# Attention before two MLPs, one core: exp of a score tile in two instructions, and products with v that end behind a turn

## The chip, the core and the metric

The kernel runs on 1 core of one Trainium2 chip. The metric is device time in microseconds (us), the median of 3 runs. TensorE is called PE here, VectorE DVE, ScalarE ACT, GpSimd POOL, and the queue that issues most transfers SP.

## The reference

Three stages follow one another; the change touches the first alone. All inputs are float32.

```python
# attention: q, k, v are (2, 8, 1152, 64)
q_pool = q.reshape(B, H, S // 2, 2, D).mean(axis=3)          # 576 queries a head
scores = scale * q_pool @ k^T                                # 576 x 1152 a head
attn   = exp(scores - max) / (sum + 1e-9)
x      = (attn @ v)  laid out as (1152 tokens, 512)
# first MLP:  h = x @ w_in;  g = P(h) / Q(h);  x = g @ w_out     (512 -> 2048 -> 512)
# second MLP: rms norm, silu(xn @ w_gate) * (xn @ w_val) @ w_out (512 -> 1536 -> 512)
```

## The kernel before, in words

**Pairs and slots.** Attention works on one head of each batch together, a *pair* `h` (8 pairs; the middle six are a loop of three rounds with two pairs each). The 1152 queries of a pair are nine *tiles* of 128 queries against 1152 keys: tiles 0 to 3 of the first batch, tile 4 mixed of both (`MIXED`), tiles 5 to 8 of the second. `pair` on each engine goes over the tiles; what PE does between two turns is called a *slot* here, slot `i` beginning with the turn of tile `i`:

- `turn(i)` (L817): nine 128x128 transposes by matmul of the probabilities, back into the PSUM buffer `sc` of the same tile, in three chunks `c` of 384 keys. It waits for the exp of tile `i` (`exp_done`).
- some `pv` matmuls (L835): the product of transposed probabilities with v, for a *group* of queries (`GROUPS`: g0 of 256 columns, g1 and g2 of 320, g3 of 256). A group takes 18 matmuls, nine key tiles for each of the two halves (high and low part) of the probabilities, `pt_hi` and `pt_lo`. `PV_AT` says which matmuls lie in which slot: (group, first, end). g3 is done in slots 0 and 1 of the next pair.
- `qk(i + 2)` (L809): the scores of the tile after next, two matmuls of 384 columns for each of three chunks, three for the mixed tile (so slot 2 has nine). Each chunk waits until DVE has taken the same chunk of tile `i` out of the buffer (`pt_lo`), since there are two buffers `sc`.

**The other engines, tile by tile.** DVE: three maxima over the chunks of tile `i + 1` (L1211), their minimum with sign (L1213), then three `lo_parts` of tile `i` (L1220), which also free `sc`. ACT: three `hi_parts` of tile `i` (L1039) as the chunks are turned, then exp of tile `i + 1` (L1030) as one instruction over 1152 elements with a sum of each row; the sum comes out by a further instruction (ACTIVATION_READ_ACCUMULATOR), and `exp_done` is counted with it. Behind the exp come, in some slots, the evacuations `o_copy` of a finished group (L1057), `sums_plus` (sum + 1e-9, L1045) in slot 0 for the pair before, and `recip_copy` in slot 3 (L1050). The reciprocal itself is on DVE in slot 2 (L1224), its turn on PE in slot 3 (L842).

**Columns.** `pt` has room for two groups; tile `i` is written into `PT_COL[i]`. `hi_parts` of tiles 0, 2, 5 and 7 open a group's columns anew and wait until the group that was there is multiplied (`pv_done`). In the kernel before, that group has ended at least one slot earlier.

**SP and POOL.** SP takes its transfers in program order: raw k and q of the next pair, `shift` (the outputs `o_sb` of the pair before to `o_part`, L385; waits for all four `o_copy`), in odd pairs `load_first_w` (weights of the first MLP), `rows_of_recip`, raw k, q, v. `o_copy(0)` of a pair waits for that `shift` to have landed. POOL splits q, k and v in high and low parts for the next pair; v of the second batch (`values_hi(1)`, L555) waits for the last group of the pair before.

Of the kernel before, what the change touches and what calls it, by code (L numbers as in the profile page):

```python
# [23 lines left out]
P = 128  # L24
# [54 lines left out]

PV_AT = {0: (3, 0, 9), 1: (3, 9, 18), 2: (0, 0, 3), 3: (0, 3, 9), 4: (0, 9, 18), 5: (1, 0, 9), 6: (1, 9, 18), 7: (2, 0, 9), 8: (2, 9, 18)}  # L80
GROUP_OF = {0: 0, 1: 0, 2: 1, 3: 1, 4: 1, 5: 2, 6: 2, 7: 3, 8: 3}


def build(nc, q, k, q_mixed, v, w_in, w_out, a, b, w_gate, w_val, w_out2, rms_g, out):
# [3 lines left out]
    with top:  # L88
# [18 lines left out]
        rms_bias = sbuf(top, "rms_bias", [P, 1])  # L107
        eps_bias = sbuf(top, "eps_bias", [P, 1])
        g_col = sbuf(top, "g_col", [P, DK])
# [7 lines left out]
        neg_part = sbuf(top, "neg_part", [P, 2, 3])  # L117
        sums = sbuf(top, "sums", [P, 2, TILES])
        sums_eps = sbuf(top, "sums_eps", [P, 2, TILES])
# [223 lines left out]
        def _(sp):  # L343
# [76 lines left out]
            def pair(h, par, n):  # L420

                if is_last(h):
                    mixed_keys(1, h)
                    shift(h - 1, 1 - par, n)
                    load_first_w(n)
                    rows_of_recip(h - 1, 1 - par)
                    last_shift(0)
                    last_rows(0)
                    last_shift(1)
                    last_rows(1)  # L430
                    last_shift(2)
                    load_w(sp, *order[0])
                    last_shift(3)
                    return
# [7 lines left out]
                if not is_first(h):  # L442
                    shift(h - 1, 1 - par, n)
                    if par == 1:
                        load_first_w(n)
                    rows_of_recip(h - 1, 1 - par)
                sp.wait_ge(k_split[1], h * 2 + 2)
# [64 lines left out]
        def _(pool):  # L512
# [5 lines left out]
            nc.gpsimd.memset(exp_bias[:], -Q_SHIFT * LN2).then_inc(consts, 1)  # L518
            nc.gpsimd.memset(eps_bias[:], 1e-9).then_inc(consts, 1)
            nc.gpsimd.memset(rms_bias[:], -0.5 * M_SHIFT * LN2).then_inc(consts, 1)  # L520
# [52 lines left out]
            def split_first_half(h):  # L573

                pool.wait_ge(k_split[1], h * 2)
                values_free(1, h - 1)
                queries_sum(0, h)
                values_hi(1)
                pool.wait_ge(q_split[0], h * 4 + 1)
                values_lo(1, h - 1)  # L580
                queries_hi(0)
                keys_hi(0)
                queries_lo(0, h)
                pool.wait_ge(q_split[0], h * 4 + 4)
                keys_lo(0, h)
# [198 lines left out]
        def _(pe):  # L784
# [27 lines left out]
            def turn(i, h, par):  # L812
                pe.wait_ge(exp_done, h * 9 + (i + 1))
                for c in range(3):
                    for j in range(3):
                        m = 3 * c + j
                        ins = nc.tensor.transpose(sc[par][:, c, P * j:P * j + P], prob[par][:, P * m:P * m + P], ident[:])  # L817
# [27 lines left out]
            def pair(h, par, n):  # L845
                for i in range(TILES):
# [10 lines left out]
                    if is_last(h) and i == 8:  # L857
# [3 lines left out]
                        first_product(0)  # L861
                    if i in (0, 1):
                        if not is_first(h):
                            g, j0, j1 = PV_AT[i]
                            pv(g, h - 1, j0, j1)
                    elif is_first(h) and i <= 4:
                        if i >= 3:
                            pv(0, h, *((0, 8) if i == 3 else (8, 2 * KEY_TILES)))
                    elif is_last(h) and i == 7:
                        pv(2, h, 0, 2 * KEY_TILES)  # L870
                    elif not (is_last(h) and i == 8):
                        g, j0, j1 = PV_AT[i]
                        pv(g, h, j0, j1)
                    if i + 2 < TILES:
# [152 lines left out]
        def _(act):  # L1027
            def exps(i, h, s):
                act.wait_ge(max_done, h * 9 + (i + 1))
                nc.scalar.activation(prob[s][:].rearrange("p (c n) -> p c n", c=3), sc[s][:, :, 0:KBANK], ACT.Exp,  # L1030
                                     bias=neg_max[:, s:s + 1], accum_out=sums[:, (s + i) % 2, i:i + 1]).then_inc(exp_done, 1)

            def hi_parts(i, h, s):
                if i in (0, 2, 5, 7) and not (is_first(h) and i < 5):
                    act.wait_ge(pv_done, h * 4 + (GROUP_OF[i] - 1))
                for c in range(3):
                    act.wait_ge(pt_t, (h * 9 + i) * 3 + c + 1)
                    src = sc[s][:, c, 0:KBANK].rearrange("p (t n) -> p t n", t=3)
                    nc.scalar.activation(pt[0][:, 3 * c:3 * c + 3, PT_COL[i]:PT_COL[i] + P], src, ACT.Copy).then_inc(pt_hi, 1)  # L1039

            def sums_plus(h, par, t0=0, t1=TILES):

                act.wait_ge(consts, 6)
                act.wait_ge(exp_done, h * 9 + t1)
                nc.scalar.activation(sums_eps[:, par, t0:t1], sums[:, par, t0:t1], ACT.Identity, bias=eps_bias[:]).then_inc(sums_done, 1)  # L1045

# [12 lines left out]
            def pair(h, par, n):  # L1059
                for i in range(TILES):  # L1060
# [8 lines left out]
                    if i == 2 and is_first(h):  # L1069
                        act.wait_ge(raw_v[0], 16)  # L1070
                        nc.scalar.activation(v2[0][:, :, 0], vraw[0][:], ACT.Copy).then_inc(v_split[0], 1)
                    if i == 1 and not is_first(h):
                        o_copy(3, h - 1)
                    if i == 0 and not is_first(h):
                        sums_plus(h - 1, 1 - par)
                    if i == 3 and not is_first(h):
                        recip_copy(0, h, 1 - par)
                    if is_last(h) and i in (3, 7):
                        sums_plus(h, par, *(SUMMED[0:2] if i == 3 else SUMMED[1:3]))
                    if is_last(h) and i == 8:  # L1080
                        recip_copy(PAIRS, PAIRS + 1, 2, *SUMMED[1:3])
                    for g in {4: [0], 6: [1], 8: [] if is_last(h) else [2]}.get(i, []):
                        o_copy(g, h)
# [44 lines left out]
            act.wait_ge(coefs, 3)  # L1128
            act.wait_ge(consts, 6)
            def square(t):  # L1130
# [73 lines left out]
        def _(dve):  # L1204
# [10 lines left out]
            def lo_parts(i, h, s):  # L1215
                for c in range(3):
# [3 lines left out]
                    nc.vector.tensor_tensor(pt[1][:, kt, col], src, pt[0][:, kt, col].bitcast(F32), ALU.subtract).then_inc(pt_lo, 1)  # L1220

            def recips(count, par, t0=0, t1=TILES):
                dve.wait_ge(sums_done, count)
# [9 lines left out]
            def pair(h, par, n):  # L1233
                for i in range(TILES):
# [195 lines left out]
```

## Time and profile before

| | us |
|---|---|
| median of 3 runs | 683.77 (683.64 to 684.41) |
| the profiled execution | 684.07 |
| its span in the trace | 682.3 |
| attention in that span | up to about 244 |
| one pair in steady state, turn of tile 0 to turn of tile 0 | 29.3 |

The page gives, for each engine, the busy time over the whole span. The three stages have different limits, so that shares of the span say little on the change; the rows below are read inside one steady pair (70.50 to 99.80 us). The starts of PE matmuls, not their durations, show its pace, because matmuls overlap. The granted clock of TensorE is at its full level (1.00) in every stretch.

### The profile page before, as it was taken

The numbers are of one execution on the slowest core, as the hardware profiler recorded it, in microseconds if no ns is written. First come the engines' busy times: TensorE is split into PE (matmuls) and PEld (weight loads), VectorE is DVE, ScalarE is ACT, GpSimd is POOL, SyncE is SP. The second block draws the span as 40 slices with busy tenths as digits, with TensorE's granted clock in tenths as the row PEclk, the third lists the DMA queues.
The fourth block names the chain that finished last, engine by engine and source line by source line (L and its number), as shares of the span: only waits on it lengthen the run. The fifth ranks groups of instructions, "written<-read, shape, count | busy, mean of one in ns | idle before, by whom it ended". The sixth has DMA issues, their size and how long they took to land.

```text
span 682.3 us, 11834 instructions
## 1 busy us (share of the span) xinstructions
PE 671.4 (98%) x3940; PEld 624.5 (92%) x3940; DVE 514.2 (75%) x1005; ACT 410.8 (60%) x861; POOL 443.4 (65%) x439
## 2 busy tenths in 40 slices
PE   8999999999999999999999999999999999999998
PEld 6899999999999999889999989899999999999996
DVE  6899999999999957989889889977554444444432
ACT  5777877888787878998888888844511111111110
POOL 5887999998999979999889789845614440000000
PEclk9999999999999999999999999999999999999999
DMA  8667467665655420101110110132111100000012
GB/s 219 198 168 203 129 178 227 181 191 149 197 150 150 114 90 0 62 24 39 62 62 5 59 62 18 45 107 80 61 63 62 62 0 1 1 0 1 1 61 78
DMA packets 26012, 60.76 MB, mean 89 GB/s; under 512 B 3304, under 2 KB 7920, under 8 KB 25840
## 3 DMA queue, kind: packets, MB, share of 16 engines
q1 hardware_dynamic: 25680, 59.87, 29.7%
q8 instruction: 25, 0.41, 0.3%
q10 hardware_dynamic: 288, 0.33, 0.2%
q14 instruction: 19, 0.16, 0.1%
HBM read 43.78 MB, written 2.40 MB: 68 GB/s over the span
## 4 chain that ended last, share of the span: by engine, by line
PE 85%; POOL 5%; DVE 4%; ACT 2%; issue 2%; DMA 1%; SPq 0%; DVEq 0%; POOLq 0%; ACTq 0%
PE hb L909 29%; PE ob L966 22%; PE sc L809 11%; PE sc L817 9%; PE misc L835 5%; PE pv_ps L835 5%; PE tb L909 3%; DVE neg_part L1211 1%; POOL num L768 1%; POOL num L766 1%; DMA qrawA<-in_q 1%; DVE pt_lo L1220 0%; ACT num L1107 0%; POOL kqB L595 0%; DVE num L1271 0%
## 5 line engine op out<-in xcount | busy, mean ns | idle before, releaser
L1039 ACT ACTIVATE pt_hi<-sc 128x384 fp32r<-128x384 f32 x216 | 90.4, 492 | 46.3 <-PE sc L817 46.3
L1211 DVE TENSOR_REDUCE neg_part<-sc 128x1 f32<-128x384 f32 x216 | 107.8, 549 | 11.2 <-PE sc L809 9.8
L1220 DVE TENSOR_TENSOR pt_lo<-sc,pt_hi 128x384 fp32r<-128x384 f32 x216 | 106.6, 548 | 2.9 <-ACT pt_hi L1039 1.9
L966 PE MATMUL ob<-wo_hi,gt_hi 128*128 128x512 f32 x252 | 99.6, 395 | 0.5 <-DVE gt_lo L1288 0.5
L966 PE MATMUL ob<-wo_lo,gt_hi 128*128 128x512 f32 x252 | 99.2, 394 | 0.0
L966 PE MATMUL ob<-wo_hi,gt_lo 128*128 128x512 f32 x252 | 99.1, 393 | 0.0
L909 PE MATMUL hb<-xt_hi,wi_hi 128*128 128x384 f32 x280 | 94.8, 339 | 1.0 <-DVE gt_lo L1288 0.7
L909 PE MATMUL hb<-xt_lo,wi_hi 128*128 128x384 f32 x280 | 94.2, 336 | 0.0
L909 PE MATMUL hb<-xt_hi,wi_lo 128*128 128x384 f32 x280 | 94.1, 336 | 0.0
L1030 ACT ACTIVATE prob<-sc,neg_max 128x1152 f32<-128x1152 f32 x72 | 89.1, 1238 | 3.1 <-DVE neg_max L1213 3.1
L817 PE MATMUL sc<-ident,prob 128*128 128x128 f32 x648 | 82.8, 273 | 0.0
L817 PEld LDWEIGHTS sc<-ident,prob 128*128 128x128 f32 x648 | 73.2, 141 | 4.5
L1177 ACT ACTIVATE silu<-hb 128x384 f32<-128x384 f32 x36 | 17.7, 490 | 93.6 <-DVE hb L1364 93.6
L766 POOL TENSOR_TENSOR num<-num,h 128x384 f32<-128x384 f32 x48 | 55.7, 1160 | 16.9 <-ACT lin L1108 16.7
L1185 ACT ACTIVATE gt_hi<-silu 128x384 fp32r<-128x384 f32 x36 | 18.9, 525 | 64.0 <-DVE silu L1369 64.0
L966 PEld LDWEIGHTS ob<-wo_lo,gt_hi 128*128 128x128 f32 x252 | 47.3, 188 | 10.8
L909 PEld LDWEIGHTS hb<-xt_hi,wi_hi 128*128 128x128 f32 x280 | 52.6, 188 | 3.7 <-issue 0.9
L966 PEld LDWEIGHTS ob<-wo_hi,gt_hi 128*128 128x128 f32 x252 | 47.3, 188 | 9.3 <-DVE gt_lo L1288 0.8
L966 PEld LDWEIGHTS ob<-wo_hi,gt_lo 128*128 128x128 f32 x252 | 47.4, 188 | 8.4
L909 PEld LDWEIGHTS hb<-xt_hi,wi_lo 128*128 128x128 f32 x280 | 52.6, 188 | 1.9
L768 POOL TENSOR_TENSOR num<-num,lin 128x384 f32<-128x384 f32 x48 | 50.4, 1050 | 3.8
L909 PEld LDWEIGHTS hb<-xt_lo,wi_hi 128*128 128x128 f32 x280 | 52.6, 188 | 0.0
(173 smaller groups left out, 1706.1 us busy)
## 6 DMA issues: line engine op xcount, KB each, us to landing
wraw<-in_moe_w_out SPq DMA_DIRECT2D x6, 1024.0 KB, 5.0
krawB<-in_k SPq DMA_DIRECT2D x8, 576.0 KB, 4.4
qrawB<-in_q SPq DMA_DIRECT2D x8, 512.0 KB, 5.7
krawA<-in_k SPq DMA_DIRECT2D x7, 576.0 KB, 4.7
o_part<-o_sb SPq DMA_DIRECT2D x14, 288.0 KB, 4.1
qrawA<-in_q SPq DMA_DIRECT2D x7, 512.0 KB, 6.1
wraw<-in_moe_w_in SPq DMA_DIRECT2D x3, 1024.0 KB, 5.0
wraw<-in_moe_w_gate SPq DMA_DIRECT2D x3, 1024.0 KB, 5.1
```

The lines of the kernel that those rows point to most:

```text
L766: nc.gpsimd.tensor_tensor(nm[:], nm[:], h2[:], ALU.mult).then_inc(num, 1)
L768: nc.gpsimd.tensor_tensor(nm[:], nm[:], ln[:], ALU.add).then_inc(num, 1)
L809: ins = nc.tensor.matmul(sc[par][:, c, 0:KBANK], lhs, rhs, start=n == 0, stop=n == len(terms) - 1)
L817: ins = nc.tensor.transpose(sc[par][:, c, P * j:P * j + P], prob[par][:, P * m:P * m + P], ident[:])
L835: ins = nc.tensor.matmul(bank[:, 0:n], v2[x][:, kt].rearrange("p a d -> p (a d)"), pt[e][:, kt, GROUP * buf + c0:GROUP * buf + c0 + n], st ...
L909: ins = nc.tensor.matmul(bank[:, 0:BLOCK], w[i][:, d, col], x[j][:, d, BLOCK * nb:BLOCK * nb + BLOCK], start=d == 0 and n == 0, stop=d == ...
L966: ins = nc.tensor.matmul(ob[(m + 1) % 2][:], gt[i][:, f, P * t:P * t + P], wo[c % 2][j][:, f, :], start=f == 0 and n == 0, stop=f == CHUNK ...
L1030: nc.scalar.activation(prob[s][:].rearrange("p (c n) -> p c n", c=3), sc[s][:, :, 0:KBANK], ACT.Exp, bias=neg_max[:, s:s + 1], accum_out=s ...
L1039: nc.scalar.activation(pt[0][:, 3 * c:3 * c + 3, PT_COL[i]:PT_COL[i] + P], src, ACT.Copy).then_inc(pt_hi, 1)
L1185: nc.scalar.activation(gt[0][:, f, BLOCK * nb:BLOCK * nb + BLOCK], silu[m % 2], ACT.Copy).then_inc(g_hi, 1)
L1211: nc.vector.tensor_reduce(neg_part[:, s, c:c + 1], sc[s][:, c, 0:KBANK], AX.X, ALU.max, negate=True).then_inc(part_done, 1)
L1220: nc.vector.tensor_tensor(pt[1][:, kt, col], src, pt[0][:, kt, col].bitcast(F32), ALU.subtract).then_inc(pt_lo, 1)
```

## The change

- `exps` becomes two ACT instructions, chunks 0 and 1 (768 elements) and chunk 2 (384), each with a sum of its own and an `exp_done` of its own (`EXP_PARTS`). `turn` waits for the first before chunk 0 and for the second before chunk 2.
- `PV_AT` is a list for each slot now, and groups end in the slot *behind* the turn of the tile that takes their columns: g2 keeps two matmuls for slot 0 of the next pair, g3 three for slot 2, g1 one for slot 7. Products in slots 0 to 8 were 9, 9, 3, 6, 9, 9, 9, 9, 9 and are 8, 9, 5, 8, 8, 9, 8, 9, 8. In `hi_parts` only the last chunk waits for `pv_done` (for tile 5 the first).
- `sums_plus` moves from ACT (slot 0) to DVE (slot 1, behind `lo_parts`), where one instruction adds both sums and 1e-9. The constant `eps_bias` and its memset go.
- `o_copy(2)` moves from slot 8 to slot 0 of the next pair, `o_copy(3)` from slot 1 to slot 2. So `shift` is due later, and `load_first_w` goes ahead of it on SP. On POOL `queries_sum(0)` goes ahead of the wait of `values_free`.

```diff
-PV_AT = {0: (3, 0, 9), 1: (3, 9, 18), 2: (0, 0, 3), 3: (0, 3, 9), 4: (0, 9, 18), 5: (1, 0, 9), 6: (1, 9, 18), 7: (2, 0, 9), 8: (2, 9, 18)}
+PV_AT = {0: ((2, 1, 16, 18), (3, 1, 0, 6)), 1: ((3, 1, 6, 15),), 2: ((3, 1, 15, 18), (0, 0, 0, 2)), 3: ((0, 0, 2, 10),), 4: ((0, 0, 10, 18),),
+         5: ((1, 0, 0, 9),), 6: ((1, 0, 9, 17),), 7: ((1, 0, 17, 18), (2, 0, 0, 8)), 8: ((2, 0, 8, 16),)}
+PV_FIRST = {0: (), 1: (), 2: (), 3: ((0, 0, 0, 8),), 4: ((0, 0, 8, 18),)}
+PV_LAST = {6: ((1, 0, 9, 18),), 7: ((2, 0, 0, 18),), 8: ()}
+EXP_PARTS = ((0, 2), (2, 3))
...
-                    shift(h - 1, 1 - par, n)
                     if par == 1:
                         load_first_w(n)
+                    shift(h - 1, 1 - par, n)
...
                 pool.wait_ge(k_split[1], h * 2)
+                queries_sum(0, h)
                 values_free(1, h - 1)
-                queries_sum(0, h)
...
             def turn(i, h, par):
-                pe.wait_ge(exp_done, h * 9 + (i + 1))
                 for c in range(3):
+                    for part, (c0, _) in enumerate(EXP_PARTS):
+                        if c == c0:
+                            pe.wait_ge(exp_done, h * 18 + (2 * i + part + 1))
...
-                nc.scalar.activation(prob[s][:].rearrange("p (c n) -> p c n", c=3), sc[s][:, :, 0:KBANK], ACT.Exp,
-                                     bias=neg_max[:, s:s + 1], accum_out=sums[:, (s + i) % 2, i:i + 1]).then_inc(exp_done, 1)
+                for part, (c0, c1) in enumerate(EXP_PARTS):
+                    dst = prob[s][:, KBANK * c0:KBANK * c1].rearrange("p (c n) -> p c n", n=KBANK)
+                    nc.scalar.activation(dst, sc[s][:, c0:c1, 0:KBANK], ACT.Exp, bias=neg_max[:, s:s + 1],
+                                         accum_out=sums[:, part, (s + i) % 2, i:i + 1]).then_inc(exp_done, 1)
...
-                if i in (0, 2, 5, 7) and not (is_first(h) and i < 5):
-                    act.wait_ge(pv_done, h * 4 + (GROUP_OF[i] - 1))
                 for c in range(3):
+                    if c == (0 if i == 5 else 2) and i in (0, 2, 5, 7) and not (is_first(h) and i < 5):
+                        act.wait_ge(pv_done, h * 4 + (GROUP_OF[i] - 1))
...
-                    if i == 1 and not is_first(h):
-                        o_copy(3, h - 1)
-                    if i == 0 and not is_first(h):
-                        sums_plus(h - 1, 1 - par)
+                    if i in (0, 2) and not is_first(h):
+                        o_copy(2 if i == 0 else 3, h - 1)
...
+            def sums_plus(h, par, t0=0, t1=TILES):
+
+                dve.wait_ge(exp_done, h * 18 + 2 * t1)
+                nc.vector.scalar_tensor_tensor(out=sums_eps[:, par, t0:t1], in0=sums[:, 0, par, t0:t1], scalar=1e-9,
+                                               in1=sums[:, 1, par, t0:t1], op0=ALU.add, op1=ALU.add).then_inc(sums_done, 1)
...
                     lo_parts(i, h, s)
+                    if i == 1 and not is_first(h):
+                        sums_plus(h - 1, 1 - par)
```

## Rows read from the trace of the kernel before

**Rows 1.** The page, first part: busy us (share of the span) and instructions

```profile
PE 671.4 (98%) x3940; PEld 624.5 (92%) x3940; DVE 514.2 (75%) x1005; ACT 410.8 (60%) x861; POOL 443.4 (65%) x439
```

**Rows 2.** Busy time by window: start:end, us, busy us and instructions of each engine, clock

```profile
core 0: us, PE busy (x) PEld busy (x) DVE busy (x) ACT busy (x) POOL busy (x), PEclk, DMA share, GB/s
70.50:86.30 15.80, 15.60 (x116) 14.62 (x115) 15.34 (x38) 12.97 (x29) 14.77 (x17) 1.00 0.47 134
86.30:99.80 13.50, 13.50 (x97) 13.29 (x97) 12.17 (x30) 10.61 (x23) 13.17 (x7) 1.00 0.70 194
```

**Rows 3.** Timeline of PE: turns of tiles 0, 1, 2, 3, 5, next 0 (start, length)

```profile
70.50 1.14 PE L817 MATMUL sc<-ident,prob 128*128 128x128 f32 x9
...
73.62 1.15 PE L817 MATMUL sc<-ident,prob 128*128 128x128 f32 x9
...
76.72 1.15 PE L817 MATMUL sc<-ident,prob 128*128 128x128 f32 x9
...
80.11 1.14 PE L817 MATMUL sc<-ident,prob 128*128 128x128 f32 x9
...
86.31 1.14 PE L817 MATMUL sc<-ident,prob 128*128 128x128 f32 x9
...
99.80 1.15 PE L817 MATMUL sc<-ident,prob 128*128 128x128 f32 x9
```

**Rows 4.** Timeline of PE: v products and scores in slots 8, 0 and 2

```profile
68.26 0.31 PE L835 MATMUL pv_ps<-pt_hi,v2B 128*128 128x320 f32 x1
...
69.43 1.23 PE L809 MATMUL sc<-kqA 128*128 128x384 f32 x6
...
71.40 0.36 PE L835 MATMUL misc<-pt_hi,v2B 128*128 128x256 f32 x1
71.61 0.28 PE L835 MATMUL misc<-pt_lo,v2B 128*128 128x256 f32 x1
...
72.56 1.22 PE L809 MATMUL sc<-kqA 128*128 128x384 f32 x6
...
78.42 0.44 PE L809 MATMUL sc<-km_hi,qm 128*128 128x384 f32 x1 [0.20 <-DVE pt_lo L1220]
```

**Rows 5.** Timeline of DVE, slots 0 and 2

```profile
69.98 1.49 DVE L1211 TENSOR_REDUCE neg_part<-sc 128x1 f32<-128x384 f32 x3 [0.28 <-PE sc L809]
...
71.58 1.48 DVE L1220 TENSOR_TENSOR pt_lo<-sc,pt_hi 128x384 fp32r<-128x384 f32 x3
...
77.82 1.47 DVE L1220 TENSOR_TENSOR pt_lo<-sc,pt_hi 128x384 fp32r<-128x384 f32 x3
79.21 0.20 DVE L1224 RECIPROCAL recip<-sums_eps 128x9 f32<-128x9 f32 x1
79.33 1.53 DVE L1211 TENSOR_REDUCE neg_part<-sc 128x1 f32<-128x384 f32 x3
```

**Rows 6.** Timeline of ACT, slot 0

```profile
71.03 1.26 ACT L1039 ACTIVATE pt_hi<-sc 128x384 fp32r<-128x384 f32 x3 [0.59 <-PE sc L817]
72.16 1.24 ACT L1030 ACTIVATE prob<-sc,neg_max 128x1152 f32<-128x1152 f32 x1
73.26 0.22 ACT L1030 ACTIVATION_READ_ACCUMULATOR prob<-sc,neg_max 128x1 f32 x1
73.35 0.32 ACT L1045 ACTIVATE sums_eps<-sums,eps_bias 128x9 f32<-128x9 f32 x1
```

**Rows 7.** Groups of ACT instructions by form: count, busy us, mean ns, idle before

```profile
L1039 ACT ACTIVATE pt_hi<-sc 128x384 fp32r<-128x384 f32 x216 | 90.4, 492 | 46.3 <-PE sc L817 46.3
L1030 ACT ACTIVATE prob<-sc,neg_max 128x1152 f32<-128x1152 f32 x72 | 89.1, 1238 | 3.1 <-DVE neg_max L1213 3.1
...
L1057 ACT ACTIVATE o_sb<-pv_ps 128x256 f32<-128x256 f32 x8 | 3.2, 403 | 0.0
L1057 ACT ACTIVATE o_sb<-pv_ps 128x320 f32<-128x320 f32 x7 | 3.2, 457 | 0.0
```

**Rows 8.** Line 385 (`shift`), 14 transfers: issue to landing

```profile
DMA to landing us min/median/max: 3.2/4.1/6.6
```

**Rows 9.** Timeline of POOL behind tile 2's turn

```profile
79.12 0.68 POOL L555 TENSOR_SCALAR v2B<-vrawB 128x576 fp32r<-128x576 f32 x1
```

More of the change, by code:

```diff
@@ L107, in build @@
         rms_bias = sbuf(top, "rms_bias", [P, 1])
-        eps_bias = sbuf(top, "eps_bias", [P, 1])
         g_col = sbuf(top, "g_col", [P, DK])
@@ L117, in build @@
         neg_part = sbuf(top, "neg_part", [P, 2, 3])
-        sums = sbuf(top, "sums", [P, 2, TILES])
+        sums = sbuf(top, "sums", [P, 2, 2, TILES])
         sums_eps = sbuf(top, "sums_eps", [P, 2, TILES])
@@ L423, in pair @@
                     mixed_keys(1, h)
+                    load_first_w(n)
                     shift(h - 1, 1 - par, n)
-                    load_first_w(n)
                     rows_of_recip(h - 1, 1 - par)
@@ L518, in _ @@
             nc.gpsimd.memset(exp_bias[:], -Q_SHIFT * LN2).then_inc(consts, 1)
-            nc.gpsimd.memset(eps_bias[:], 1e-9).then_inc(consts, 1)
             nc.gpsimd.memset(rms_bias[:], -0.5 * M_SHIFT * LN2).then_inc(consts, 1)
@@ L861, in pair @@
                         first_product(0)
[L862 to L873, printed above, removed]
+                    special = PV_FIRST if is_first(h) else PV_LAST if is_last(h) else {}
+                    for g, back, j0, j1 in special.get(i, PV_AT[i]):
+                        pv(g, h - back, j0, j1)
                     if i + 2 < TILES:
@@ L1039, in hi_parts @@
                     nc.scalar.activation(pt[0][:, 3 * c:3 * c + 3, PT_COL[i]:PT_COL[i] + P], src, ACT.Copy).then_inc(pt_hi, 1)
[L1041 to L1045, printed above, removed]
             def recip_copy(n, count, slot, t0=0, t1=TILES):
@@ L1071, in pair @@
                         nc.scalar.activation(v2[0][:, :, 0], vraw[0][:], ACT.Copy).then_inc(v_split[0], 1)
-                    if i == 1 and not is_first(h):
-                        o_copy(3, h - 1)
-                    if i == 0 and not is_first(h):
-                        sums_plus(h - 1, 1 - par)
+                    if i in (0, 2) and not is_first(h):
+                        o_copy(2 if i == 0 else 3, h - 1)
                     if i == 3 and not is_first(h):
                         recip_copy(0, h, 1 - par)
-                    if is_last(h) and i in (3, 7):
-                        sums_plus(h, par, *(SUMMED[0:2] if i == 3 else SUMMED[1:3]))
                     if is_last(h) and i == 8:
                         recip_copy(PAIRS, PAIRS + 1, 2, *SUMMED[1:3])
-                    for g in {4: [0], 6: [1], 8: [] if is_last(h) else [2]}.get(i, []):
+                    for g in {4: [0], 6: [1]}.get(i, []):
                         o_copy(g, h)
@@ L1128, in _ @@
             act.wait_ge(coefs, 3)
-            act.wait_ge(consts, 6)
+            act.wait_ge(consts, 5)
             def square(t):
@@ L1240, in pair @@
                     if is_last(h) and i == 8:
+                        sums_plus(h, par, *SUMMED[1:3])
                         coefficients()
@@ L1246, in pair @@
                     if is_last(h) and i == 4:
+                        sums_plus(h, par, *SUMMED[0:2])
                         recips(PAIRS, par, *SUMMED[0:2])
```

## The prediction, made before the change was run

> **What bounds the kernel now.** First the busy times [rows 1]: PE 98% of the span, DVE 75%, ACT 60%. That is an average over three stages, and the change lives in the first. So next the windows of one steady pair [rows 2]. In the second, slots 5 to 8, PE is busy for all 13.50 us, DVE for 12.17. In the first, slots 0 to 4, PE is busy for 15.60 of 15.80 and DVE for 15.34: two engines near their limit. ACT has room in both.
>
> Then the turns on PE's timeline [rows 3]. Slots 0, 1 and 2 last 3.12, 3.10 and 3.39 us, slots 3 and 4 together 6.20, slots 5 to 8 together 13.49 (3.37 each). The pair takes 29.30.
>
> PE's own pace comes from starts of matmuls [rows 3, 4]. A turn takes 71.40 - 70.50 = 0.90. The first v product behind it takes 0.21, each further one (72.56 - 71.61) / 8 = 0.119 with 256 columns and (69.43 - 68.26) / 8 = 0.146 with 320. Six score matmuls take 73.62 - 72.56 = 1.06. So a slot with nine narrow products needs 0.90 + 0.21 + 8 x 0.119 + 1.06 = 3.12, which is just what slot 0 takes, and one with nine wide products 0.90 + 0.21 + 8 x 0.146 + 1.06 = 3.34 against 3.37. **In seven of nine slots PE has no gap worth closing.** It loses time in slot 2, where its three products are over at 76.72 + 0.90 + 0.21 + 2 x 0.119 = 78.07 and the mixed tile's scores start at 78.42, waiting for DVE's `pt_lo` [rows 4]: 0.35. In slots 3 and 4 its own work is 6.0 (2.88 with six products and the reciprocal's turn, which I count as one more transpose, 0.10 to 0.11; 3.12 with nine) against 6.20: 0.2.
>
> **The exp alone.** Now a turn waits for the whole exp. It starts 73.26 - 72.16 = 1.10 before the read of its sum, and that read takes 0.22 [rows 6]: 1.32, and some 0.05 for the signal. From two copies [rows 7] an element costs (457 - 403) / 64 = 0.84 ns, so the exp's fixed part is 1238 - 0.84 x 1152 = 270 ns: 0.92 us for 768 elements, 0.59 for 384. The other end is the line through the 384-element copy and the exp, 0.97 ns an element: 0.87 and 0.49. I take the first, since fixed parts belong to the operation. With the overlap of 0.14 that the exp shows (1.24 long, next at 1.10) the first part's signal comes at 0.78 + 0.22 = 1.00, or 0.32 earlier than now, the second's at 0.78 + 0.09 + 0.45 + 0.22 = 1.54, later by 0.22, but chunk 2 is turned 0.60 behind chunk 0. ACT is kept for 0.78 + 0.09 + 0.45 + 0.09 = 1.41 instead of 1.19. That 0.22 a tile lies in ACT's idle time before `hi_parts` (0.59 in slot 0). So this edit by itself moves nothing in slots whose turn follows the scores without a gap, and has a little to give in slot 3 only.
>
> The Trainium skill, "ScalarE: Activation LUTs", section "What ACT_TABLE_LOAD costs", gives an activation with a pointer as bias 280 ns and 0.833 ns an element, back-to-back ones overlapping by some 93 ns. By that the parts are 0.92 and 0.60, and the trace agrees at 1152 elements: 1.24.
>
> **Products moved.** Slots 5 to 8 held 36 wide products and hold 34: 2 x 0.146 = 0.29 less. They are PE's alone, DVE has slack there, and slots 6 and 8 at 3.37 - 0.15 = 3.22 stay above what DVE needs for a tile: 1.60 from maxima to `pt_lo` (69.98 to 71.58) and 1.39 on to the next (77.82 to 79.21), 2.99 [rows 5]. So 0.29 a pair is gained in full.
>
> Slots 0 to 4 get those two and lose none of their own. PE alone would need, in slots 0, 1, 2, 3 and 4, 3.03, 3.12, 3.17, 3.12 and 3.01: 15.45 against 15.81 now. But DVE and the latency decide:
> - Slot 0. Two wide products of g2 stand behind the turn; they end at about 0.90 + 0.21 + 0.31 = 1.42 behind the turn's start, with the signal 1.5. The last `hi_parts` chunk would start at 0.53 + 2 x 0.385 = 1.30 [rows 6], so it is 0.2 late, its `pt_lo` chunk hardly (due at 71.58 + 0.93, or 2.01 behind the turn; ready at 2.04). The slot comes to 3.09.
> - ACT then: exp from 1.89, free at 3.30, `o_copy(2)` for 0.37 to 3.67, when `hi_parts` of tile 1 could start at 3.09 + 0.53 = 3.62. A tie: 0 to 0.15 late, I take 0.03.
> - Slot 1. `sums_plus` on DVE: between 0.07 (near nothing beside its neighbours) and 0.25 (its 0.32 on ACT, in full); I take 0.12, what the reciprocal takes between its start and the next maxima [rows 5]. With M0 for the turn of tile 0, `pt_lo` of tile 1 starts at M0 + 3.67 + 0.53 = 4.20 and DVE reaches the next maxima at 4.20 + 1.39 + 0.12 = 5.71. Now it does so at 5.72, held by PE. So it is covered, with nothing left over: each further 0.1 costs 0.1.
> - Slot 2. The mixed scores start when DVE has freed chunk 0, at M0 + 5.72 + 1.60 + 0.60 = M0 + 7.92 as now (0.60: 77.82 to 78.42). The two more products fill the hole. The turn of tile 3 stays at M0 + 9.61.
> - Slots 3 and 4: 3.12 (eight products, no hole) and 3.09, the loop from the turn over `pt_lo` back to the scores' last chunk: 1.08 to `pt_lo` (70.50 to 71.58), 1.48 for its three chunks, 0.06 signal, 0.12 weights, 0.35 for two matmuls. Together 6.21, now 6.20.
>
> So slots 0 to 4 stay at 15.8, and **the whole gain is the 0.29 of slots 5 to 8**.
>
> **What else moves.** `queries_sum(0)` now runs on POOL while g3 ends at about 76.72 + 1.5 = 78.3; v is split at 79.12 [rows 9], so that wait stays covered, by 0.8. `shift` is issued some 3.5 us later (two transfers, behind `load_first_w` in odd pairs). In pair 0 and the last the lists for slots of their own hold as many products as before; the last `sums_plus` and reciprocal lie under 18 products of slot 7. Startup stays: its turns are held by `pt_lo` too. What attention gains, the MLPs pass on, since POOL's first chain there starts from PE's first unit.
>
> **Sum.** Pairs 0 to 6: 7 x 0.29 = 2.05. Less 7 x 0.01 and 6 x 0.03: 1.8. The profiled execution took 684.07 (span 682.3, 1.8 around it), 0.30 above the median. 684.07 - 1.8 = 682.27, and from the median 683.77 - 1.8 = 682.0.
>
> **Rivals.**
> 1. *DVE and ACT take it back.* `sums_plus` at 0.25 costs 0.13 a pair, the late `hi_parts` of tile 1 up to 0.15, a late last chunk in slots 0 and 2 the rest. For it: both engines tie with PE in slot 1. Gain 0 to 1.3: 682.5 to 683.8.
> 2. *PE's floor.* The holes close too: 29.30 - (15.45 + 13.20) = 0.65 a pair, 6 x 0.65 + 0.29 = 4.2, so 679.6; closed in part, 680 to 681. It needs PE's holes to hang on exp. Against it: the row says `pt_lo`. The Trainium skill, "Perfetto Trace Analysis", section "Optimizing Scalar/DVE Operations", says that breaking up instructions of engines that aren't saturated can end bubbles elsewhere sooner; by it the sum would be this rival's, and the trace agrees for slot 3 at most.
> 3. *Slower: `o_copy(0)` waits for `shift`.* `o_copy(3)` ends near M0 + 6.21 + 3.65, so the second transfer is issued at 10.4. ACT comes to `o_copy(0)` at M0 + 12.7 + 3.07 = 15.8. It decides from a landing of 5.4 on; now landings take 3.2 to 6.6, median 4.1 [rows 8]. At 6.6 ACT stalls by 1.2, less 0.24 of slack, and PE has no slack in slot 5: 1.0 a pair. In all four odd pairs that is 4 - 1.8 = 2.2 more: 686.0. Against it: `shift` then follows the raw k, q and weights by 3 us instead of running among them.
>
> **How the numbers follow.** A measurement of this kernel can tell about 0.2%, 1.4 us, from no change. Forecast 60%, its own range 681.2 to 683.0, of which three quarters lie below 682.4; rival 1 22%, rival 2 9%, rival 3 9%. Faster by over 0.2%: 0.45 + 0.09 = 0.54; slower: rival 3 and some mishap, 0.08; the rest, 0.38, within. The range reaches from the near part of rival 2 past the end of rival 1: 680.8 to 684.0.
>
> **What would show it.** Slots 6 and 8 of a steady pair at 3.22, slots 5 and 7 still at 3.37, the pair at 29.0 to 29.1. The mixed scores start 7.9 behind the turn of tile 0, waiting for `pt_lo`, PE's hole there 0.1 instead of 0.35. Exp at 0.92 and 0.59. ACT's idle before `hi_parts` near zero in slot 1. The forecast is wrong if slots 0 to 4 come out away from 15.8 by more than 0.15, or if ACT waits for a transfer in slot 4.

## The result, and the profile after

| | before | after |
|---|---|---|
| median, us | 683.92 (683.64 to 684.41, 4 runs) | 692.99 (692.1 to 693.57, 4 runs) |
| the profiled execution, and its span | 684.07, 682.3 | 692.1, 690.3 |
| first matmul of the first MLP to the last matmul | 244.15 to 678.59: 434.44 | 249.60 to 686.65: 437.04 |

The ratio is 1.0129 [1.0117, 1.0141]: the change costs 1.3% where 0.25% of gain was forecast. The profiled executions differ by 8.0 us, of which 5.45 lie ahead of the first MLP and 2.6 in the MLPs, which the change does not touch. The granted clock is 1.00 in both.

The page after, its first part as in [rows 1]:

```profile
PE 675.1 (98%) x3940; PEld 625.0 (91%) x3940; DVE 515.5 (75%) x1014; ACT 427.5 (62%) x996; POOL 443.3 (64%) x438
```

PE, with as many instructions, is busy for 3.7 us more, and 4.3 us more of the span lie outside its busy time. The groups by form, as in [rows 7]:

```profile
L1027 ACT ACTIVATE prob<-sc,neg_max 128x768 f32<-128x768 f32 x72 | 66.0, 916 | 2.4 <-DVE neg_max L1200 2.4
L1027 ACT ACTIVATE prob<-sc,neg_max 128x384 f32<-128x384 f32 x72 | 43.3, 601 | 0.0
L1212 DVE SCALAR_TENSOR_TENSOR sums_eps<-sums 128x9 f32<-128x9 f32 x7 | 3.7, 534 | 0.0
L1048 ACT ACTIVATE o_sb<-misc 128x320 f32<-128x320 f32 x8 | 3.5, 440 | 9.3 <-PE misc L839 9.3
```

The exp costs ACT 109.3 us instead of 89.1, as forecast. Two of these rows are odd. `sums_plus` takes 534 ns on average for nine elements a row. And ACT stood idle for 9.3 us in front of the copies of 320 columns out of `misc`, where it waited for nothing before:

```profile
L1057 ACT ACTIVATE o_sb<-misc 128x320 f32<-128x320 f32 x8 | 3.7, 458 | 0.0
```

The windows of the pair that [rows 2] shows, slots 0 to 4 and slots 5 to 8 (the columns are the same):

```profile
70.69:86.75 16.06, 15.84 (x118) 15.07 (x117) 15.73 (x39) 14.18 (x39) 15.02 (x18) 1.00 0.44 127
86.75:100.70 13.95, 13.62 (x95) 12.86 (x94) 12.18 (x29) 11.51 (x32) 13.47 (x8) 1.00 0.68 195
```

The second window, PE's own where DVE has slack, grew from 13.50 to 13.95 although it holds two products fewer, and PE has a hole of 0.33 in it. Slot by slot, from the starts of the turns (as in [rows 3]; us, the last column to the next turn of tile 0):

```
slot               0     1     2     3     4     5     6     7     8    pair
before, pair 2   3.11  3.10  3.39  3.05  3.15  3.37  3.37  3.37  3.38  29.30
after,  pair 2   3.15  3.10  3.64  3.09  3.08  3.35  3.22  4.17  3.21  30.01
before, pair 4   3.11  3.11  3.38  3.05  3.14  3.35  3.34  3.37  3.37  29.23
after,  pair 4   3.14  3.11  4.28  3.09  3.08  3.34  3.22  4.17  3.22  30.65
```

Slots 6 and 8 are the 3.22 of the forecast. Slot 7 is 4.17 or 4.18 in each of pairs 0 to 6, and slot 2 is long in pairs 2, 4, 6 and 7 only. PE's timeline of slot 7 of pair 2, from the end of slot 6 to the turn of tile 8 (start, length):

```profile
92.25 1.23 PE L811 MATMUL sc<-kqB 128*128 128x384 f32 x6
93.33 1.14 PE L821 MATMUL sc<-ident,prob 128*128 128x128 f32 x9
94.22 0.39 PE L839 MATMUL misc<-pt_lo,v2A 128*128 128x320 f32 x1
94.45 0.30 PE L839 MATMUL pv_ps<-pt_hi,v2B 128*128 128x320 f32 x1
...
95.47 0.31 PE L839 MATMUL pv_ps<-pt_lo,v2B 128*128 128x320 f32 x1
96.11 1.54 PE L811 MATMUL sc<-kqA 128*128 128x384 f32 x6 [0.33 <-DVE pt_lo L1207]
97.49 1.14 PE L821 MATMUL sc<-ident,prob 128*128 128x128 f32 x9
```

The single product into `misc` behind the turn of tile 7 is g1's last. The scores of slot 7 could have started at 95.62, one step of 0.146 after the last product; they start at 96.11, and then last 1.38 to the next turn instead of 1.06: 0.49 + 0.32 = 0.81, the growth of the slot. PE waits for `pt_lo`; what was late ahead of that is on ACT's timeline (the first two lines are of slot 0, for the comparison further down):

```profile
72.63 0.90 ACT L1027 ACTIVATE prob<-sc,neg_max 128x768 f32<-128x768 f32 x1
...
74.38 0.89 ACT L1036 ACTIVATE pt_hi<-sc 128x384 fp32r<-128x384 f32 x2
...
91.76 0.92 ACT L1027 ACTIVATE prob<-sc,neg_max 128x768 f32<-128x768 f32 x1
...
92.63 0.60 ACT L1027 ACTIVATE prob<-sc,neg_max 128x384 f32<-128x384 f32 x1
...
94.65 0.44 ACT L1048 ACTIVATE o_sb<-misc 128x320 f32<-128x320 f32 x1 [1.32 <-PE misc L839]
94.98 1.25 ACT L1036 ACTIVATE pt_hi<-sc 128x384 fp32r<-128x384 f32 x3
96.09 0.93 ACT L1027 ACTIVATE prob<-sc,neg_max 128x768 f32<-128x768 f32 x1
```

ACT stands still for 1.32 us in front of `o_copy(1)`, which waits for g1's last product. Behind it in ACT's program are the `hi_parts` of tile 7: due 0.53 behind their turn (93.86), they start at 94.98. The `exp` of tile 8 is behind those. The chain of waits (start, length, what), with `issue` and queue steps between, names the same steps in order:

```profile
93.49 0.98 PE sc L821 x9
94.47 0.16 PE misc L839
...
94.65 0.04 ACT o_sb L1048
...
94.99 0.49 ACT pt_hi L1036
...
95.50 0.57 DVE pt_lo L1207
...
96.11 1.54 PE sc L811 x6
```

Among the waits from 20 to 246 us this one stands third, with its count of 7: once in each pair but the last (in total, times, longest).

```profile
ACT pt_hi L1036 <- PE sc L821: 21.3, 44, 1.7
PEld sc L811 <- DVE pt_lo L1207: 10.0, 33, 1.1
ACT o_sb L1048 <- PE misc L839: 9.3, 7, 1.3
```

The second loss is in slots 1 and 2. The timeline of pair 4, all engines:

```profile
135.89 1.30 POOL L661 TENSOR_TENSOR wo_lo<-wout_raw,wo_hi 128x512 fp32r<-128x512 f32 x1
...
136.11 1.11 DVE L1212 SCALAR_TENSOR_TENSOR sums_eps<-sums 128x9 f32<-128x9 f32 x1
...
137.14 1.47 DVE L1198 TENSOR_REDUCE neg_part<-sc 128x1 f32<-128x384 f32 x3
...
139.22 1.42 POOL L561 TENSOR_TENSOR v2B<-vrawB,v2B 128x576 fp32r<-128x576 f32 x1
...
139.33 0.45 PE L811 MATMUL sc<-km_hi,qm 128*128 128x384 f32 x1 [0.87 <-DVE pt_lo L1207]
...
140.12 0.20 DVE L1217 RECIPROCAL recip<-sums_eps 128x9 f32<-128x9 f32 x1
```

`sums_plus`, nine elements a row, takes 1.11 us here, and ends at 137.22 with the POOL instruction beside it (137.19). In pair 2 it takes 0.47, from 76.32, and again ends with the POOL instruction beside it (L659, to 76.78). In pairs 1 and 3 it takes 0.16: in pair 1 POOL runs nothing beside it, in pair 3 a POOL instruction starts at the same moment, 106.33, and runs to 106.81 without holding it. So in these pairs it depends on what POOL has begun when DVE comes. The reciprocal on the same engine, under POOL's L561, takes its usual 0.20. PE is idle for 0.87 ahead of the mixed scores; before it was 0.20, and in pairs 1, 3 and 5, where `sums_plus` takes 0.16, it is not idle there at all.

The sum of the 5.45: slot 7, 7 x 0.80 = 5.6; slots 6 and 8, about -2.0; slots held by `sums_plus`, 0.25 + 0.90 + 0.89 + 0.32 in slot 2 of pairs 2, 4, 6 and 7 and 0.23 in slot 5 of the last, 2.6; the part ahead of pair 1 without its slots 6 to 8, -0.8. Together 5.4. The last term need not be the change's: the turn of tile 0 of pair 1 starts at 41.26 before, but at 40.42 in e2 below, whose attention is the same program.

The third loss is in the MLPs. In PE's timeline of the second MLP, the start of one product of twelve matmuls (`wi`) and of the next (`wv`), both times in the second of its three chunks of weights (the buffers `wi1` and `wv1`), before:

```profile
547.05 0.34 PE L909 MATMUL hb<-xt_hi,wi_hi 128*128 128x384 f32 x1
...
549.13 0.34 PE L909 MATMUL hb<-xt_hi,wv_hi 128*128 128x384 f32 x1
```

and after:

```profile
535.79 0.34 PE L904 MATMUL hb<-xt_hi,wi_hi 128*128 128x384 f32 x1
...
537.91 0.34 PE L904 MATMUL hb<-xt_hi,wv_hi 128*128 128x384 f32 x1
```

Twelve matmuls in 2.08 us and in 2.12, that is 0.1733 and 0.1767 each, without a wait between them. This part of the program is the same in both kernels. What differs is where its buffers lie: `sums` has a second plane (72 bytes a partition more) and `eps_bias` is gone. If buffers are laid out in steps of 32 bytes, all that are allocated behind `sums` lie 32 bytes further on. No run prints an address; the places below are worked out by this rule, and e2, e9 and e12 were built by it and came out as it says.

### The profile page after: what moved, and what is told of

It is laid out like the page before. It is cut to its first block, busy times and chain, and to the rows that moved or that the text cites. A ratio compares the mean times of both kernels' runs of the same rounds, so it can differ in the third digit from the quotient of the medians.

```text
span 690.3 us, 12027 instructions
## 1 busy us (share of the span) xinstructions
PE 675.1 (98%) x3940; PEld 625.0 (91%) x3940; DVE 515.5 (75%) x1014; ACT 427.5 (62%) x996; POOL 443.3 (64%) x438
## 4 chain that ended last, share of the span: by engine, by line
PE 83%; DVE 6%; POOL 5%; ACT 3%; issue 2%; DMA 1%; SPq 0%; ACTq 0%; DVEq 0%; POOLq 0%
PE hb L904 29%; PE ob L961 22%; PE sc L811 11%; PE sc L821 9%; PE misc L839 4%; PE pv_ps L839 4%; PE tb L904 3%; DVE pt_lo L1207 2%; DVE neg_part L1198 2%; POOL num L770 1%; POOL num L768 1%; DMA qrawA<-in_q 1%; ACT pt_hi L1036 0%; ACT num L1094 0%; POOL kqB L597 0%
## 5 line engine op out<-in xcount | busy, mean ns | idle before, releaser
L1036 ACT ACTIVATE pt_hi<-sc 128x384 fp32r<-128x384 f32 x216 | 92.0, 494 | 26.5 <-PE sc L821 22.9
L1027 ACT ACTIVATE prob<-sc,neg_max 128x768 f32<-128x768 f32 (+1 forms) x144 | 106.3, 759 | 2.4 <-DVE neg_max L1200 2.4
L821 PEld LDWEIGHTS sc<-ident,prob 128*128 128x128 f32 x648 | 75.1, 141 | 3.2 <-issue 0.8
```

Of the source, the lines that this page charges most:

```text
L1027: nc.scalar.activation(dst, sc[s][:, c0:c1, 0:KBANK], ACT.Exp, bias=neg_max[:, s:s + 1], accum_out=sums[:, part, (s + i) % 2, i:i + 1]).th ...
```

## The experiments

Three theories were put to the test, each on one of the losses. **A**: `o_copy(1)`, left in ACT's slot 6 while its last product moved into PE's slot 7, holds ACT. **B**: `sums_plus` is held by POOL because it reads two inputs from SBUF; **B2**, formed when that fell: `scalar_tensor_tensor` and `tensor_scalar` from SBUF to SBUF are held, `tensor_reduce` and `reciprocal` are not. **C**: the MLPs' matmuls are slower because of their buffers' addresses; its rival is that the MLPs inherit something from attention's end.

**e1.** The change, with g1's copy in ACT's slot 7.

```diff
-                    for g in {4: [0], 6: [1]}.get(i, []):
+                    for g in {4: [0], (6 if is_last(h) else 7): [1]}.get(i, []):
```

> The changed kernel with one edit: ACT copies group g1 out behind the exp of slot 7 instead of slot 6 (in the last pair, where g1 still ends in slot 6, as it is). Theory A, the copy of g1 stands in front of the matmul that it waits for: slot 7 falls from 4.17 to 3.37 us in all seven pairs, 7 x 0.8 = 5.6 us less, some 687.4 us. Rival, the second exp instruction or the two late matmuls behind the turn make slot 7 long: slot 7 stays above 3.9 and the time at 693.

688.77 (688.56 to 689.48), ratio to before 1.0076 [1.0059, 1.0092]. Slot 7 is 3.34 to 3.37 in pairs 0 to 6, and pairs without a held `sums_plus` take 28.96 to 29.0. ACT's timeline of slots 6 and 7 (the turn of tile 7 of pair 2 is at 92.37, 0.96 earlier than in the changed kernel):

```profile
92.89 1.38 ACT L1036 ACTIVATE pt_hi<-sc 128x384 fp32r<-128x384 f32 x3 [0.52 <-PE sc L821]
94.16 0.90 ACT L1027 ACTIVATE prob<-sc,neg_max 128x768 f32<-128x768 f32 x1
...
95.03 0.58 ACT L1027 ACTIVATE prob<-sc,neg_max 128x384 f32<-128x384 f32 x1
...
95.59 0.44 ACT L1048 ACTIVATE o_sb<-misc 128x320 f32<-128x320 f32 x1
```

`hi_parts` of tile 7 start 0.52 behind the turn, and the copy comes behind the exp without a wait: A is shown. The gain is 4.2 and not 5.6, because the pairs now meet POOL elsewhere: `sums_plus` takes 0.59, 1.24, 0.59 and 0.97 in pairs 4 to 7 and 1.26 behind tile 4 of the last, and slot 2 of these pairs takes 3.78, 4.42, 3.77 and 4.19. In all it costs some 3.4 instead of 2.6. The MLPs take 437.48, 0.4 more. What one loss costs depends on the other.

**e2.** The kernel before, with 32 unused bytes behind `sums`.

```diff
         sums = sbuf(top, "sums", [P, 2, TILES])
+        sbuf(top, "pad", [P, 8])
```

> The kernel before with one unused buffer of 32 bytes behind `sums`, which moves all later SBUF buffers by the 32 bytes by which the change moves them. Theory C, the addresses of the weights set the pace of 384-column matmuls in the MLPs (0.1734 us from one to the next before, 0.1767 after, only where the weights lie in buffers that moved): 2.5 us slower than before, 686.4, with 0.1767 in the products from the second weight buffers. Rival, a drift of that one execution: the time stays at 683.9.

686.13 (685.38 to 686.33), ratio 1.0034 [1.0020, 1.0049], not one instruction changed. The MLPs take 436.75 instead of 434.44, at 0.1767 for the matmuls that took 0.1733. This is C, and it speaks against its rival, since attention is the one of before. In numbers: 432 matmuls on `wv` and as many on `wi1`, up to 0.0034 more each, are up to 2.9 us, and the MLPs took 2.3 more here and 2.6 in the changed kernel.

**e3.** The changed kernel with the same 32 bytes more.

> The changed kernel with 32 unused bytes behind `sums`, so that the later buffers lie 64 bytes from where they lay before. Theory C: the MLPs get their 2.5 us back, 690.5 us. Rival, drift or the number of instructions before the MLPs: 693.

692.31 (692.1 to 692.97), 1.0127 [1.0110, 1.0144]. The matmuls on `wv` are back at 0.1733 to 0.1737 and the MLPs at 435.88, 1.2 less than without the bytes, but `sums_plus` was held in five pairs in this run (slot 2 of 4.28, 3.54, 4.27, 4.29 and 3.67), so that little of it shows in the time.

**e4.** The changed kernel, with one sum read instead of two. The sum over the last 384 keys is left out of the denominator.

```diff
-                nc.vector.scalar_tensor_tensor(out=sums_eps[:, par, t0:t1], in0=sums[:, 0, par, t0:t1], scalar=1e-9,
-                                               in1=sums[:, 1, par, t0:t1], op0=ALU.add, op1=ALU.add).then_inc(sums_done, 1)
+                nc.vector.tensor_scalar(sums_eps[:, par, t0:t1], sums[:, 0, par, t0:t1], 1e-9, None, ALU.add).then_inc(sums_done, 1)
```

> The changed kernel with `sums_plus` on DVE reading only the first sum (one SBUF input instead of two; the sum of the last 384 keys is left out of the denominator). Theory B, the instruction with two SBUF inputs is held while GpSimd has the port (1.11 us instead of 0.16 in pairs 4 and 6, 0.47 in pair 2, 0.58 in pair 7): it takes 0.1 to 0.2 everywhere, slot 2 is 3.39 in all pairs, 2.1 to 2.7 us less, some 690.6. Rival, it waits for the second exp part or for the sums: slot 2 of pairs 4 and 6 stays at 4.27 and the time at 693.

693.45 (692.57 to 693.7), 1.0138 [1.0121, 1.0155]. The timeline of pair 4:

```profile
136.78 1.30 POOL L661 TENSOR_TENSOR wo_lo<-wout_raw,wo_hi 128x512 fp32r<-128x512 f32 x1
...
136.98 1.13 DVE L1212 TENSOR_SCALAR sums_eps<-sums 128x9 f32<-128x9 f32 x1
```

With one input it is held just as long, ending at 138.11 beside POOL's 138.08. B fell as it stood: no second input is needed for the hold. Whether the second input is what holds `scalar_tensor_tensor` is not shown, since the form changed with it. The Trainium skill, "SBUF — State Buffer", section "SBUF: two separate sides", describes a port pair shared by VectorE and GpSimd as an exclusive lock that a VectorE instruction takes in a two-port performance mode or, against a GpSimd instruction that reads SBUF, with two SBUF inputs; the loser is blocked for the whole instruction. By it both forms can be held, and the trace agrees for both.

**e5.** e1, with the sums added by a reduction over three planes; the third holds 1e-9, written once.

```diff
-        sums = sbuf(top, "sums", [P, 2, 2, TILES])
+        sums = sbuf(top, "sums", [P, 3, 2, TILES])
...
+            nc.gpsimd.memset(sums[:, 2], 1e-9).then_inc(consts, 1)
...
+                nc.vector.tensor_reduce(sums_eps[:, par, t0:t1], sums[:, :, par, t0:t1].rearrange("p e t -> p t e"), AX.X, ALU.add).then_inc(sums_done, 1)
```

> The changed kernel with the copy of g1 behind slot 7's exp, and with `sums_plus` on DVE as one tensor_reduce over three parts (both sums and a constant part of 1e-9). Theory B2: what is held beside GpSimd is a DVE instruction of the forms scalar_tensor_tensor or tensor_scalar from SBUF to SBUF, while tensor_reduce and reciprocal never were (0.16 and 0.20 in every trace). It takes under 0.25 in all pairs, slot 2 is 3.39 everywhere, 3 to 3.6 us less than the 688.8 of the same kernel with scalar_tensor_tensor: 685.4. Rival, any small DVE instruction at that point is held (the place matters, not the form): instructions of 0.6 to 1.2 us remain and the time stays at 688.8.

684.48 (683.83 to 685.28), ratio to 683.68 1.0010 [0.9998, 1.0022]. The timeline of pair 4:

```profile
132.43 0.61 POOL L660 TENSOR_SCALAR wo_hi<-wout_raw 128x512 fp32r<-128x512 f32 x1
...
132.51 0.17 DVE L1214 TENSOR_REDUCE sums_eps<-sums 128x9 f32<-128x27 f32 x1
```

It ends at 132.68, under a POOL instruction that runs to 133.04, the `wo_hi` one that held `sums_plus` in pair 2 of the changed kernel. Behind tile 4 of the last pair it takes 0.16 from 229.11, under the `wo_lo` one (228.58 to 229.87) of the kind that held it for 1.11. In all pairs it takes 0.16 to 0.18, in pairs 1 to 6 slot 2 takes 3.38 or 3.39, and a pair 28.98 to 29.02: B2. Attention is over at 241.42, of which 1.3 lie ahead of pair 1, which starts at 39.92 here and at 41.26 before. The buffers of the MLPs now lie 96 bytes further than before, and the MLPs take 437.23.

**e6.** e5 with 32 bytes more, 128 in all. The idea was that a shift by a multiple of 64 is free.

> The same with 32 unused bytes, so that the second weight buffers lie as before, modulo 64 bytes. Theory: all three costs are gone and what is left is the forecast's gain of 0.29 a pair in slots 5 to 8: 682 to 683 us, faster than before. Rival, the moved products and the second exp give nothing net: 684.

686.85 (685.38 to 688.6), 1.0050 [1.0034, 1.0065]. Pairs as in e5, MLPs at 437.90 and the matmuls at 0.1769. The idea fell: the matmuls on `wv` have their old pace at 64 bytes (e3) and their slowest at 128.

**e7.** The kernel before with nothing but the exp in two and the sums on DVE by the reduction, addresses as in e6.

```diff
-                pe.wait_ge(exp_done, h * 9 + (i + 1))
                 for c in range(3):
+                    for part, (c0, _) in enumerate(EXP_PARTS):
+                        if c == c0:
+                            pe.wait_ge(exp_done, h * 18 + (2 * i + part + 1))
```

> The kernel before with the exp in two instructions alone (sums added by a tensor_reduce on DVE in slot 1, 32 unused bytes so that later buffers lie as before modulo 64 bytes); products, copies and queues as before. Forecast's step: the exp alone moves nothing in slots without a gap, 683.0 to 684.2, slots 5 to 8 at 3.37, ACT's exp 0.92 and 0.60. Rival, it shortens the wait before the mixed tile's scores or the slots behind it: 682.5 or less.

687.71 (687.3 to 690.14), 1.0064 [1.0050, 1.0077]. The pair stays at 29.19 to 29.25, slots 5 to 8 at 3.37, slot 4 at 3.11 against 3.15, the first MLP starts at 244.38 against 244.15, and the MLPs take 438.07. The split exp by itself gives attention next to nothing, and 3.6 of the 4.0 lost are in the MLPs, whose program is the same: the loss of the addresses. The rule cited in the prediction from the Trainium skill, "Perfetto Trace Analysis", section "Optimizing Scalar/DVE Operations", that breaking up instructions can end bubbles elsewhere sooner, finds 0.04 in slot 4 here and nothing else.

**e8.** The other half: products, copies (g1's in slot 7) and queue order of the change, one exp, `sums_plus` on ACT in slot 1, addresses as before.

> The changed kernel's products, column waits, copies of g2 and g3 and queue order, with one exp instruction and `sums_plus` on ACT as before (now in slot 1, since slot 0 has the copy of g2), and the copy of g1 in slot 7; buffers as before. By the forecast's numbers the exp of tile 1 starts 0.2 later in slot 0 and its end decides the next turn: slot 0 at 3.30 instead of 3.12, slots 6 and 8 at 3.22, net 0.1 a pair less: 683 us. If the two-part exp is what makes the moved products pay, this one is no better than before (683.8) while the one with both is at 682 to 683. Rival, the second exp instruction isn't needed: this one is as fast as the one with both.

683.56 (682.74 to 686.27), 1.0000 [0.9991, 1.0009]. ACT's timeline of slot 0:

```profile
70.94 0.87 ACT L1033 ACTIVATE pt_hi<-sc 128x384 fp32r<-128x384 f32 x2 [0.78 <-PE sc L820]
71.97 0.49 ACT L1033 ACTIVATE pt_hi<-sc 128x384 fp32r<-128x384 f32 x1 [0.15 <-PE pv_ps L838]
72.35 1.22 ACT L1024 ACTIVATE prob<-sc,neg_max 128x1152 f32<-128x1152 f32 x1
```

Slots 6 and 8 take 3.23, but slot 0 takes 3.30 and the pair 29.24 to 29.27. The last chunk of `hi_parts` waits for g2's two products, the whole exp behind it starts at 72.35 and its sum is out at 73.66, and the turn of tile 1 starts at 73.71. So the products alone give nothing either: what slots 6 and 8 gain, slot 0 loses, unless the turn can start on the first part of the exp. The two halves need each other.

**e9.** All three losses undone: g1's copy in slot 7, the reduction, and `sums` allocated behind attention's other buffers, with placeholders so that every other buffer lies where it lay before.

```diff
+        sbuf(top, "pad0", [P, 1])
...
-        sums = sbuf(top, "sums", [P, 2, 2, TILES])
+        sbuf(top, "pad", [P, 2 * TILES])
...
         wout_raw = sbuf(att, "wout_raw", [P, D])
+        sums = sbuf(att, "sums", [P, 3, 2, TILES])
```

> The changed kernel with the copy of g1 in slot 7, `sums_plus` as a tensor_reduce, and the enlarged `sums` put behind the attention's other buffers, so that every other buffer has exactly the address that it has in the kernel before. Theory, the forecast's sum holds once the three costs are gone: pairs of 29.0 us, 1.8 us less in attention, and the MLPs at their 434.4 to 434.8: 681.5 to 682.3, faster. Rival, the MLPs' pace hangs on something else than addresses (number of instructions ahead, chip): they stay near 437 and the time at 684.5.

682.98 (682.16 to 683.62, 11 runs) against 684.16: ratio 0.9984 [0.9975, 0.9993], faster than both kernels, if only by 1.2 us than the one before. (That is above the 682.3 that was expected at most.) Slots of a steady pair: 3.15, 3.11, 3.38, 3.08, 3.09, 3.35, 3.20, 3.35, 3.20, together 28.91 to 29.00. Its windows of slots 0 to 4 and 5 to 8, from the turns of tiles 0 and 5 of pair 2 and the next turn of tile 0 (70.03, 85.86, 99.02):

```profile
70.03:85.86 15.83, 15.83 (x118) 15.08 (x117) 15.48 (x39) 14.21 (x39) 14.79 (x18) 1.00 0.44 128
85.86:99.02 13.16, 13.16 (x95) 13.01 (x94) 12.14 (x29) 11.68 (x32) 12.83 (x7) 1.00 0.71 208
```

PE is busy in all of both. Slots 0 to 4 take 15.81 to 15.84 in pairs 1 to 6, where they took 15.78 to 15.81, and slots 5 to 8 take 13.09 to 13.16, where they took 13.43 to 13.50. The mixed scores start 7.95 to 7.97 behind the turn of tile 0, without idle time of PE in front. The first MLP starts at 242.33, 1.8 earlier than before, and the MLPs take 434.74.

**e10.** The kernel before, with 32 unused bytes ahead of `wi1`, the second buffer of the MLPs' first weights, so that only what lies behind it moves.

```diff
+        sbuf(mlp, "pad", [P, 8])
         wi = [wi0, [sbuf(mlp, ...
```

> The kernel before with 32 unused bytes just ahead of `wi1`, so that only wi1, wv0, wo1, tok and rrow move, and wv1, gt and all of attention stay. Theory, the matmul's pace hangs on the address of its own stationary operand: products from wi1 and wv0 go from 0.1735 to 0.1767 us, those from wv1 stay at 0.1733; some 1.5 us slower than before, 685.2. Rival, it hangs on another buffer that is written or read meanwhile (gt, temporaries): no difference, 683.7.

686.81 (686.13 to 688.46), 1.0045 [1.0030, 1.0061]. The MLPs take 437.29, more than e2's 436.75, with attention's buffers in place. The val products take 0.1767, 0.1740 and 0.1767 in their three chunks, which lie in `wv0`, `wv1` and `wv0`; those on `wi1` take 0.1750 and not the 0.1767 that was expected. The largest share is in matmuls that the expectation did not name: the 512-column ones on `wo1`, from one start to the next, take 0.2330 on average instead of 0.2275, and there are 324 of them, 1.8 of the 2.85 us. In e2, where `gt`, their other operand, moved along with `wo1`, they take 0.2276. So each buffer's place counts, but not in a way that one rule foretold.

**e11.** The kernel before with 64 unused bytes behind `sums`.

> The kernel before with 64 unused bytes behind `sums`. Theory of a period of 64 bytes: second weight buffers at 0.1735, 683.7. Rival, no such period (the changed kernel with 128 bytes more showed 0.1769): 0.176 or more, 685 to 687.

685.41 (684.75 to 688.62), 1.0024 [1.0012, 1.0035]; val products at 0.1733 to 0.1737, MLPs at 436.17. It is as in e3, which lies at the same place with the changed attention. The MLPs are still 1.7 longer than before: in both runs the matmuls on `wo1` take 0.2305 instead of 0.2275, and those on `wo0` 0.2338 instead of 0.2329.

**e12.** The changed kernel as it is, with only `sums` moved, as in e9.

> The changed kernel as it is, but `sums` behind the attention's buffers, so that every other buffer lies where it lies before. Theory C: the MLPs take 434.5 us as before instead of 437.0, 690.5. Rival, the pace follows the program and not the addresses: 693.

691.72 (690.46 to 692.0), 1.0107 [1.0092, 1.0123]. MLPs at 435.15, slot 7 at 4.18 and slot 2 at 4.44, 3.64, 4.31, 4.30 and 3.80 in the held pairs: of the three losses one is gone and two stand. `sums_plus` is held for 1.27 in pair 2 and costs some 3.7 in all, which is why the time is above the 690.5 that was expected.

The MLPs against the place of their buffers, across all kernels:

```
bytes beyond before   kernels               val matmul, us     MLPs, us
0                     before, e8, e9, e12   0.1733 to 0.1736   434.44 to 435.15
32                    after, e1, e2, e4     0.1767, 0.1768     436.75 to 437.48
64                    e3, e11               0.1733 to 0.1737   435.88 to 436.17
96                    e5                    0.1758             437.23
128                   e6, e7                0.1769             437.90 to 438.07
```

Kernels with quite different attentions agree wherever the place agrees, to 0.7 us in the MLPs. The val matmuls are not the whole of it: at 64 bytes they have the old pace, and the MLPs are 1.4 to 1.7 longer.

## Why the prediction was wrong

It said 682.0 (680.8 to 684.0), with 0.08 for slower; it came out at 693.0. Three costs stand between the two, 5.6 us in slot 7, 2.6 at `sums_plus` and 2.6 in the MLPs, together 10.8. By its own steps:

- **The exp alone.** Right. Its parts take 0.916 and 0.601 us (0.92 and 0.59 were forecast), `exps` of tile 1 starts 1.94 behind the turn of tile 0 (1.89), and e7 shows that it moves next to nothing by itself (0.04 in slot 4).
- **Products moved, slots 5 to 8.** The size was right, 3.22 in slots 6 and 8. **This is the step that failed.** It said of the products of slots 5 to 8 "They are PE's alone", counted g1's last one in slot 7 as 0.146 of PE's time and did not ask who waits for it. The prediction checked `hi_parts` against `pv_done` where groups g2 and g3 end late, but not `o_copy(1)`, which stays in ACT's slot 6, in front of the `hi_parts` of tile 7. In [rows 6] `hi_parts` follow the turn by 0.53, while the product ends 1.28 behind it (94.61): the copy could not be ready in time. It costs 0.80 a pair, 5.6 in all. With the copy one slot later (e1, e5, e9) the step holds: 3.20 to 3.37 in slots 5 to 8.
- **Slots 0 to 4 stay at 15.8.** Right where `sums_plus` is not held: 15.81 to 15.84 in e9, with `hi_parts` of tile 1 at 3.69 behind the turn (3.67) in the changed kernel. e8's slot 0 of 3.30 shows why the split exp is needed for it.
- **`sums_plus` at 0.07 to 0.25.** Wrong, 0.16 to 1.11. The bounds came from how long it took on ACT and from a reciprocal on DVE; neither form is held by POOL. The step's own sentence, that each further 0.1 costs 0.1, held. From its start to the next maxima it takes the 0.12 of the sum where it is not held; in pair 4 it takes 0.91 more, and slot 2 grew by 0.90; in pair 2 it takes 0.28 more, and slot 2 grew by 0.25.
- **What attention gains, the MLPs pass on.** They do, but they also took 2.6 us for the 32 bytes, which no step of the prediction had in it.
- **The rivals.** Rival 1 had the right place (slot 1, DVE) and a price of 0.13 instead of up to 0.90. Rival 2 did not come: in e9 PE has no idle time left in the two windows, and the pair is at 28.9 to 29.0, not at 28.65: slots 0 to 4 did not shrink. Rival 3, the slower one, did not come; the place where ACT waited was slot 6, for a product, and not slot 4 for `shift`.

The 1.8 forecast for attention is what e9 gives (first MLP 1.8 earlier), and its median lies 1.2 below before, within the prediction's range. So what moving the products gains was priced rightly, and what the same edit sets off on ACT, on DVE and in the layout was not.

What stays open: which rule ties a buffer's place to the pace of the matmuls. The table is not monotonic, and e10 shows that `wi1`, `wv0`, `wv1` and `wo1` answer differently to the same 32 bytes. The runs show which forms are held, and that their ends coincide with POOL's; that what they wait for is a port is not shown by them.

## What to carry to other kernels

When a producer is moved by one slot, go through all who wait for its semaphore, and for each ask what stands behind the waiting instruction in its engine's program; a copy of 0.44 us cost 0.80 a pair by what it stood in front of. A tiny instruction that moves to another engine takes a new neighbour with it: price it from the same form beside that neighbour, not from its size. And if a buffer in the middle of the layout changes its size, compare an untouched stage of both traces, or keep the addresses, before a difference is put down to the schedule.

## What was not expected of the hardware

- The same matmuls, 384 columns in fp32r, without waits, run at 0.1733 or at 0.1767 us each by the place of their buffers in SBUF; those with 512 columns on `wo1` at 0.2275 to 0.2330. 32 unused bytes made a kernel 0.34% slower (e2), and over 434 us of MLPs the places tried cost 1.4 to 3.6 us.
- A DVE instruction over nine elements a row takes 0.16 to 1.27 us (e12): `scalar_tensor_tensor` and `tensor_scalar` from SBUF to SBUF can last until the POOL instruction that began before them ends, while `tensor_reduce` (0.16 to 0.18) and `reciprocal` (0.17 to 0.21) were held in none of the runs, under the same POOL instructions.
